# A five-group slot softmax, w2b loaded in pieces, seven homes for w1b and halved w2b work in the token loop of an attention and mixture-of-experts kernel

## The reference

```python
# retention attention: B, H, S, D = 4, 8, 768, 64
state = gamma * state + k_t v_t^T          # per head
y_t = q_t state / sqrt(D)                  # x = y as 3072 tokens x 512
# soft MoE: phi 512 x 32 (8 experts x 4 slots), w1 8 x 512 x 1024, w2 8 x 1024 x 512
logits = x @ phi
d = softmax(logits, over the 3072 tokens)  # slot softmax
slot_out[e] = relu((d.T @ x)[e] @ w1[e]) @ w2[e]
x = softmax(logits, over the 32 slots) @ slot_out
# top-2 MoE with noisy gates, 8 experts, w1 8 x 512 x 1024, w2 8 x 1024 x 512
top2 = the two largest of x @ w_gate + log1p(exp(x @ w_noise)) * noise
out = sum over the two experts of weight * (relu(x @ w1[e]) @ w2[e])
```

## Time and profile before

| what | value |
|---|---|
| runs | 612.53 us median of 3 (611.92, 612.53, 617.91) |
| the profiled execution | 616.65 us |
| its span on the core | 614.8 us |
| mean granted TensorE clock in it | 0.927 of full speed |
| busy: PE, PEld | 526.9 us (86%), 311.7 us (51%) |
| busy: DVE, ACT, POOL | 276.5 us (45%), 191.5 us (31%), 251.1 us (41%) |
| read from HBM, written to it | 93.87 MB, 29.70 MB |

### The profile page before, as it was taken

One profiled execution on the slowest core, in us unless ns is written; L12 is line 12 of the kernel. 1 busy time (PEld: TensorE's weight loads), 2 busy tenths in 40 slices (PEclk: granted clock), 3 DMA queues, 4 the chain that ended last, 5 costly groups with the idle time before them and its releaser, 6 DMA issues.

```text
span 614.8 us, 13368 instructions
## 1 busy us (share of the span) xinstructions
PE 526.9 (86%) x4842; PEld 311.7 (51%) x4843; DVE 276.5 (45%) x427; ACT 191.5 (31%) x349; POOL 251.1 (41%) x218
## 2 busy tenths in 40 slices
PE   4987989897875565567898999999999999999992
PEld 3866777775444542333444554555455445455451
DVE  2544646554553049883769323333332333332330
ACT  0121111222362043566695222222222222222120
POOL 1221212122010000234755766666666666666553
PEclk9998979999798656686999999999999999999997
DMA  7797897895999999883720222212232331433410
GB/s 236 261 314 277 301 321 250 307 346 205 333 378 385 388 408 405 333 324 98 289 71 22 55 51 50 44 38 48 42 52 48 47 53 24 52 49 42 52 18 1
DMA packets 48804, 107.88 MB, mean 175 GB/s; under 512 B 11482, under 2 KB 12746, under 8 KB 48769
## 3 DMA queue, kind: packets, MB, share of 16 engines
q1 hardware_dynamic: 34512, 92.89, 41.9%
q0 software_dynamic: 14256, 14.49, 13.6%
HBM read 93.87 MB, written 29.70 MB: 201 GB/s over the span
## 4 chain that ended last, share of the span: by engine, by line
PE 56%; DMA 15%; POOL 8%; issue 8%; DVE 6%; ACT 4%; SPq 0%; DVEq 0%; POOLq 0%; ACTq 0%
PE ps L859 30%; DMA w_region<-moe_w 5%; POOL out L537 4%; PE ps L570 4%; PE ps L614 4%; DMA s_region<-moe_w 3%; PE ps L609 3%; PE ps L842 3%; DMA w_region<-chunks 2%; PE ps L600 2%; POOL out L531 2%; DMA sw_region<-chunks 2%; POOL rec_region L525 2%; PE ps L714 2%; PE ps L621 2%
## 5 line engine op out<-in xcount | busy, mean ns | idle before, releaser
L859 PE MATMUL ps<-w_region,s_region 128*128 x1320 | 296.2, 381 | 1.2 <-ACT s_region L1033 1.2
L859 PEld LDWEIGHTS ps<-w_region,s_region 128*128 128x128 f16 x1320 | 127.5, 98 | 145.9 <-issue 4.8
L1432 DVE SCALAR_TENSOR_TENSOR s_region<-ps,s_region 128x1024 f16<-128x1024 f32 x55 | 67.3, 1224 | 186.3 <-ACT s_region L1033 186.3
L1033 ACT ACTIVATE s_region<-ps 128x1024 f16<-128x1024 f32 x55 | 56.2, 1023 | 71.3 <-PE ps L842 71.3
L537 POOL DMA_INDIRECT out<-s_region,rec_region x42 | 69.5, 1655 | 15.1 <-issue 12.2
L531 POOL DMA_INDIRECT out<-s_region,rec_region x42 | 47.4, 1128 | 65.7 <-DVE s_region L1446 65.4
L525 POOL DMA_INDIRECT rec_region<-records,idx x55 | 57.7, 1049 | 16.9 <-issue 16.9
L1023 ACT ACTIVATE s_region<-rec_region 128x128 f16 (+1 forms) x55 | 16.9, 307 | 129.9 <-DMA rec_region<-records,idx 129.9
L501 POOL PARTITION_ALL_REDUCE w2b_sum<-w2b_sum x8 | 8.4, 1053 | 82.6 <-ACT sw_region L953 55.9
L467 POOL TENSOR_TENSOR s_region<-w_region,s_region 128x512 f32<-128x512 f32 x14 | 15.0, 1070 | 64.2 <-DMA w_region<-chunks 45.8
L1446 DVE TENSOR_SCALAR s_region<-ps,rec_region,y_scale 128x512 f32<-128x512 f32 x42 | 33.8, 806 | 6.7 <-PE ps L859 4.0
...
## 6 DMA issues: line engine op xcount, KB each, us to landing
...
out<-s_region,rec_region POOLq DMA_INDIRECT x84, 2.8
```

The costliest lines, as they stand in the source:

```text
L859: last = nc.tensor.matmul(bank[6 + r], h[:, r, f, :], w2b_parts[:, bass.ds(e, 1), part, f, :].rearrange("p e m -> p (e m)"), start=(first ...
L1033: nc.scalar.activation(h_hi[:, r, :, :].rearrange("p c t -> p (c t)").rearrange("p (a n) -> p a n", a=2), ps[:, 2 + 2 * r:4 + 2 * r, :], A ...
L1432: nc.vector.scalar_tensor_tensor(out=h_lo[:, r, :, :].rearrange("p c t -> p (c t)").rearrange("p (a n) -> p a n", a=2), in0=ps[:, 2 + 2 * ...
```

## The change

- The slot softmax has NG = 5 groups of chunks: 0-3, 4-7, 8-13, 14-19 and 20-23. The first three are worked inside the attention, at chunks 7, 11 and 17. The fourth's products stand behind the last chunk, in PE's gaps while the last group's maximum is found. The last group has buffers of its own.
- w2b0 is loaded as three quarters (behind the last `keep_x_t`) and one quarter. w2b1 is loaded as two outer quarters (behind the fourth group's sums) and an inner half (behind the last group's).
- w1b2 goes to unit 7, and w1b now has homes in units 3 to 7 so that a load waits for an older product. w2b2 is loaded behind w1b1, w2b3 behind w1b3. w2b3 waits for `sw_product(2)`; w2b7 is loaded ahead of w2b6 and waits for w2b2's low part, w2b6 for w2b3's.
- `sw_product`s 1, 4 and 5 stand earlier on PE. On DVE the records' weights are computed behind the ranks, w2b2's scale stands later, and one low half stands ahead of the loop's last preparations where three stood. On POOL two fetches stand ahead of the second `sw_all_sum`.
- ACT makes w2b3's high part in two halves: one directly ahead of the loop, one behind `stage_c(2)`. In the loop, sums and high parts of w2b4 to w2b7 are dealt out in pieces; DVE's low parts of w2b2 (second half) and w2b3 stand behind tiles 0 and 1, of w2b4 to w2b7 behind tiles 2, 4, 5 and 6.

```diff
+    GROUPS = ((0, 4), (4, 8), (8, 14), (14, NT - REP), (NT - REP, NT))
...
-        w1b_home = [unit(u) for u in (6, 3, 4, 5, 6, 4, 5, 6)]
+        w1b_home = [unit(u) for u in (6, 3, 7, 4, 5, 6, 3, 4)]
...
                 elif e == 3:
-                    sp.wait_ge(w2b_lo_ready, 2)
+
+                    sp.wait_ge(ring_used, 2 * E + 3)
                 elif e < 6:
 
-                    sp.wait_ge(ring_used, 2 * E + e + 3)
+                    sp.wait_ge(ring_used, 2 * E + e + 1)
                 else:
-                    sp.wait_ge(w2b_lo_ready, 4)
+                    sp.wait_ge(w2b_lo_ready, {6: 4, 7: 3}[e])
...
+            sp.wait_ge(x_t_ready, NT)
+            load_w2b_quarters(0, 0, 3)
+            sp.wait_ge(slot_in_done, NG - 1)
+            load_w2b_quarters(1, 0, 1)
+            load_w2b_quarters(1, 3, 4)
+            sp.wait_ge(logits_kept, NT)
+            load_w2b_quarters(0, 3, 4)
+            sp.wait_ge(slot_in_done, NG)
+            load_w2b_quarters(1, 1, 3)
...
+            slot_sums(NG - 2, range(REP), bank[0], GROUPS[NG - 2][1])
+            turn_max(NG - 1)
+            slot_sums(NG - 2, range(REP, GROUPS[NG - 2][1] - GROUPS[NG - 2][0]), bank[0], GROUPS[NG - 2][1])
+            den_sums(NG - 2, NT)
+            spread_max(NG - 1)
+            slot_sums(NG - 1, range(REP), bank[1], NT)
...
+            w2b_high_half(3, 0)
...
-            w2b_low(2)
-            w2b_low(3, (0,))
+            w2b_low(2, (0,))
             sw_scales(1)
...
-                if i == 0:
-                    w2b_low(3, (1,))
+                if i < 2:
+                    w2b_low(*((2, (1,)), (3,))[i])
...
-                if i in (1, 3, 5, 6):
-                    w2b_low({1: 4, 3: 5, 5: 6, 6: 7}[i])
+                if i in (2, 4, 5, 6):
+                    w2b_low({2: 4, 4: 5, 5: 6, 6: 7}[i])
```

More of the change, by code:

```diff
@@ L578, in logit_parts_of @@
                     pe.wait_ge(logits_kept, b * NC + c)
-                if b > 0 and c == 3:
-                    pe.wait_ge(den_kept, b)
+                for g in group_ending(b * NC + c - 3):
+                    if g < NG - 2:
+                        pe.wait_ge(den_kept, g + 1)
                 for d in range(DC):
@@ L595, in turn_x @@
                     pe.wait_ge(x_kept, b * NC + c)
-                if b > 0 and c == 3:
-                    pe.wait_ge(slot_in_kept, b)
+                for g in group_ending(b * NC + c - 3):
+                    if g < NG - 2:
+                        pe.wait_ge(slot_in_kept, g + 1)
                 for d in range(DC):
@@ L802, in _ @@
             sw_product(0)
+            sw_product(1)
             pe.wait_ge(chosen_ready, 1)
@@ L812, in _ @@
             pe.wait_ge(ranks_read, 1)
+            sw_product(4)
             sort_rows(0)
@@ L816, in _ @@
             sw_spread_parts(1)
-            sw_product(4)
             sort_rows(1)
             sort_rows(2)
+            sw_product(5)
             sw_spread_parts(2)
             sw_spread_parts(3)
-            for e in range(5, E):
-                sw_product(e)
+            sw_product(6)
+            sw_product(7)
             for e in range(4, E):
@@ L946, in w2b_sums, with exp_slots @@
[L946 to L954 removed]
+            def exp_slots(g):
+                act.wait_ge(cols_shifted, g + 1)
+                if g > 0:
+                    nc.scalar.activation(fade[:, g:g + 1], max_all[:, g:g + 1], ACT.Exp, scale=-1.0,
+                                         bias=max_all[:, g - 1:g]).then_inc(fade_ready, 1)
+                nc.scalar.activation(exp_of(g), exp_of(g), ACT.Exp).then_inc(exp_cols_ready, 1)
@@ new lines, in keep_den @@
+            def keep_den(g):
+                act.wait_ge(den_done, g + 1)
+                nc.scalar.activation(den_part[:, g, :], bank[LG][:, 480:482], ACT.Copy).then_inc(den_kept, 1)
+            for t in range(NT):
+                keep_chunk(t)
+                for g in group_ending(t - 1):
+                    exp_slots(g)
+                for g in group_ending(t - 2):
+                    if g < NG - 2:
+                        keep_den(g)
+            keep_den(NG - 2)
+            exp_slots(NG - 1)
@@ new lines, in _, with w2b_high_half @@
+            keep_den(NG - 1)
+            def w2b_high_half(e, half):
+                if half == 0:
+                    act.wait_ge(w2b_scale_ready, e + 1)
+                    if e <= EARLY:
+                        act.wait_ge(ring_used, (4, 6, E + 5, 2 * E + 7, 3 * E)[e])
+                    else:
+                        act.wait_ge(w2b_lo_ready, e)
+                chunks = slice(half * FC // 2, (half + 1) * FC // 2)
+                nc.scalar.activation(w2b_parts[:, e, 0, chunks, :],
+                                     w2b_in[e].rearrange("p (c m) -> p c m", c=FC)[:, chunks, :],
+                                     ACT.Copy, scale=w2b_scale[:, 2, e:e + 1]).then_inc(w2b_hi_ready, 1)
@@ new lines, in w2b_high, with w2b_sum_part @@
+            def w2b_high(e):
+                for half in range(2):
+                    w2b_high_half(e, half)
+            def w2b_sum_part(e, part, unused):
+                parts, done = w2b_sum_parts(e), w2b_sums_of(e) + part
+                if part == 0:
+                    act.wait_ge(w2b_full[e], {0: 32, 1: 48}.get(e, 16))
+                if done > 0:
+                    act.wait_ge(w2b_sum_ready, done)
+                nc.scalar.activation(unused, w2b_in[e][:, part * UNIT // parts:(part + 1) * UNIT // parts], ACT.Abs,
+                                     accum_out=w2b_sum[:, 0, e, part:part + 1]).then_inc(w2b_sum_ready, 1)
@@ L956, in sw_sums @@
+            def w2b_sums(e, unused):
+                for part in range(w2b_sum_parts(e)):
+                    w2b_sum_part(e, part, unused)
             def sw_sums(e):
@@ L1389, in _ @@
             sw_scales(0)
+            w2b_scale_by_sum(2)
             by_lo = [P, LO_PART, P]
```

271 lines of the change are left out of this document (137 added, 134 removed).

## The result

| | before | after |
|---|---|---|
| median of the runs, us | 612.22 (610.51 to 617.91, 4 runs) | 624.11 (619.14 to 624.86, 4 runs) |
| ratio, 95% interval | | 1.0151 [1.0098, 1.0204] |
| profiled execution / its span | 616.65 / 614.8 | 624.86 / 623.1 |
| last product with w2a starts | 212.42 | 207.47 |
| loop's first product starts | 281.69 | 280.43 |

The change costs 1.5%. It was forecast at 614.0, no change. The weights' stream did come 5.0 us earlier, but the stretch from there to the loop became 3.7 us longer and the loop lost another 9.6.

What follows compares the result with a forecast made beforehand. The token loop was taken as the last bound, with the weights' stream holding the stages ahead. Of 4.4 us gained only 0.4 survived the late load; +1.9 behind it gave +1.5: 614.0 us against 612.53, range 608.5 to 619.0.

Steps and rivals of the forecast that it cites:

- Groups in attention: Attention's slot sums on PE: two groups need one round instead of two, gaining 1.0 us (0 to 1.9).
- The stream: Weight loads behind attention: w2b0 issued 1.8 us earlier, and 1.4 us of lost transfer rate recovered.
- Gating and folding: Stretch from the last w2a product towards the loop: 1.1 us more gained, bounds 0 and 3.
- Half high part ahead of `stage_c(0)`: Half of w2b3's high part on ACT directly ahead of the loop: costs 0.9 us (0 to 1.95).
- The loop's first tiles: w2b6 issued 8.1 us later in the loop, so its wait leaves only 0.4 of the 4.4 us gained.
- S': Start of the loop's first product in the changed kernel: forecast 277.3, 4.4 us earlier than before.
- Behind that: Tiles after the w2b6 wait: 2.0 us lost to crowded ACT, 1.7 to w2b7's wait, 1.8 saved: +1.9.
- The prediction's own sign of being wrong: Wrong if ACT's w2b6 sum doesn't wait for a DMA, the loop isn't 3 to 6 us earlier, or attention ends later.
- (a): Rival: the front ahead of the loop gains more, every bound at its good end: 611.1 us; chance 0.18.
- (d): Rival: the early loads bring nothing, as the queue's rate sets w2a's arrival: 617.2 us; chance 0.06.
- (b): Rival: the late w2b6 load holds nobody in the loop's first tiles: 606.5 us; chance 0.10.
- (c): Rival: slower because shorter slot sums leave attention's chunk loads uncovered: 620 us; chance 0.11.

Runs made afterwards that it cites:

- e4: e1 with ACT's high part of w2b2 moved behind four keeps: ratio 0.9934 to the kernel before.
- e1: Changed kernel with DVE's low parts early, w2b2's whole ahead of the loop and w2b3's behind tile 0: 616.01 us, ratio 1.0030 to the kernel before.
- e2: Changed kernel with w2b3's load issued behind w1b4 instead of w1b3: 622.22 us, ratio 1.0135 to the kernel before.
- a0: Control: the changed kernel with only one wait of PE written another way: 621.23 us, ratio 1.0111 to the kernel before.
- g2: g1 with w2b3's load issued behind that of w1b4: 605.57 us, ratio 0.9810 to the kernel before.
- b1: Kernel before with only the changed kernel's order of DVE's low parts of w2b2 and w2b3: ratio 1.0174 to the kernel before.
- e6: e1 with w2b2's high part behind four keeps, `sw_high` ahead of w2b3's sums, and the half high part behind `stage_c(2)`: ratio 0.9919 to the kernel before.
- e3: Changed kernel with both edits, w2b3's load behind w1b4 and the low parts of w2b2 and w2b3 early: 613.32 us, ratio 0.9987 to the kernel before.
- f1: e1 with w2b0 and w2b1 each loaded by one DMA instead of early pieces: 618.12 us, ratio 1.0029 to the kernel before.
- g1: e6 with both halves of w2b3's low part right behind `h_low(0)` on DVE: 606.82 us, ratio 0.9894 to the kernel before.
- e5: e1 with `sw_high` moved ahead of the sums of w2b3 on ACT: ratio 0.9976 to the kernel before.
- b0: Control: the kernel before with only one wait of PE written another way: ratio 1.0010 to the kernel before.

## Why the prediction was wrong, step by step

*Groups in attention*, 1.0 forecast. Attention ended 2.7 us earlier in the pair of profiles. But it ended at 148.45, 144.81 and 143.97 in three profiles with the old part and between 140.46 and 145.71 in twelve with the new one. The means differ by 2.1, less than either scatters: they point the forecast's way, but the gain isn't settled.

*The stream*, 1.8 + 1.4. From the end of attention to the last w2a product the old part took 63.1 to 64.1 us in three profiles, the new one 60.2 to 61.8 in eleven: 2.7 in place of 3.2. Right. The gap was closed only in part (273 GB/s from 156 to 162), because w2a's first load waits for its home and not for the queue: SP issues it at 158.36, as the product with w1a0 ends. Together the last w2a product came at 207.47, forecast 208.2.

*Gating and folding*, "-1.1" within 0 to 3. **This step failed first, by its sign.** The stretch to `sw_product(7)` grew by 2.9 us. That is no chance of one pair: it is 55.0 to 55.6 us in the three profiles with the old order, and 57.9 to 60.3 in the eight that keep both the changed part and the place of w2b3's load. I had asked "is w1b7 there?", and answered by ten units at the full 406 GB/s. I didn't ask whether SP would be allowed to issue them: the new wait of w2b3's load for `sw_product(2)` stands in front of the last four of w1b on SP and leaves the queue at 327 and 189 GB/s for 11 us. And I credited ACT with the pieces that it lost, not with those that it got: the high part of w2b2 now stands ahead of the keeps. The two costs lay beside each other. e4 took ACT's away and left the way to `sw_product(7)` at 58.0 (e1 58.2); e2 took the queue's away and left 57.1 (changed kernel 57.9, a0 60.3), because `sw_high` then stood behind the later w2b3; g2, with both gone, cut it by 4.4. And DVE's low parts, which I had counted among the pieces that leave this stretch, cost nothing there: b1 took two halves away and the loop started at the same time.

*Half high part ahead of `stage_c(0)`*, +0.9. From `sw_product(7)` to the loop it was 15.0 us, 14.3 before, with 1.8 of a stall that isn't its doing. e6 moved the half piece, and the same way took 11.7 us, but no run did that alone. Bounds kept, size open.

*The loop's first tiles.* The mechanism was right and is shown from both sides (e1, b1): issue forecast at S' + 19.8, measured 20.3; sum forecast to wait 7.6, measured 9.75. The mis-sized term is **the landing of a single load, 8.4 forecast, 10.9 measured** (10.2 to 10.3 in a0 and e2, 9.6 to 10.0 in e1, e3 to e6 and f1, 10.5 in g1). My rows were of loads into a quiet or a weights-only machine; here the records' fetches and the output rows run beside it, and in the changed kernel, a0 and e2 w2b7's load was issued only 7.8 us before. That one of these is the cause is my guess; no run was aimed at it, and g1's 10.5 came without w2b7's load beside it. The upper end of the range, 11.0, had it. The Trainium skill, DMA: Bandwidth & Descriptors, section Anatomy of one DMA, fits its fixed cost and its rate to transfers issued from GpSimd, and these are issued from SP; the estimate of 6.8 us by its figures lies further from every one of these loads than 8.4 does.

*Behind that*, 2.0 and 1.7 forecast, 1.59 and 1.67 measured: right. Not forecast was the lower clock behind the long wait, 1.5 us.

The prediction's own sign of being wrong came true: S' was to be 3 to 6 us earlier and is 1.3 earlier, and the stretches at 273, 327 and 189 GB/s lie under the 340 that it had named. The sum was +1.5, the profile has +8.3. Of the 6.8 between them 3.9 are the middle's (+3.7 for -0.2, and 1.8 of it is the stall below), 2.5 the turn's (33.5 us behind the loop's first product for 30.95), 1.5 the clock's, less 0.8 that the front gave in addition and 0.3 of the two small waits. Of the rivals, (a) and (d) fell: the front gained about what was forecast, no more and no less. (b) fell by the turn's wait. (c) named the right side with the wrong mechanism; attention never got slower. What I missed is a rival on the weights' queue: a new wait on SP in the middle of the stream.

## What to carry to other kernels

When a list of loads is re-ordered, check for each load what its queue waits for before it, and what stands behind it; bandwidth times bytes is only the time if nothing in front waits. An edit that tries out a suspected cost and brings nothing shows only that another chain is as long, or that the edit lengthened one itself: look at what now waits, and repeat it once that is cut (e2 against g2). And a piece of work whose end frees a home belongs as early as its engine has a gap, here 4.6 us of work in 6.2 us of idle time, which took 2.9 us off the span in one pair of profiles (e6 and g1; their ratios, 0.9919 and 0.9894, don't tell them apart by themselves).

## What the runs showed that wasn't expected

- The same wait gives two different tiles behind it. After PE waits of 8.79 to 10.34 us the next 24 products took 6.88 to 7.18 us in all four profiles. After 2.73 to 3.59 us they took 5.34 in four profiles (before, e3, e4, e6), but after 2.81 to 4.02 us 6.79 to 7.69 in four others (e1, e5, f1, b0), with the granted clock at 0.74 in e1's window from 302 to 308.5. A short wait can cost 1.5 to 2.3 us more than its length, and one profile doesn't tell whether it will.
- In eight of fifteen profiles PE's wait for `h_high(0)` ahead of the loop's first product was 2.4 to 4.6 us, in seven 0.8 to 1.2. The order of the instructions isn't what decides it: a0 and the changed kernel differ in one wait's form and show 1.20 and 2.98. ACT's idle time there is put down to nothing on this core ("remote"):

```profile
279.16 1.02 ACT L1092 ACTIVATE s_region<-ps 128x1024 f16<-128x1024 f32 x1 [2.96 <-remote]
```

  The products that it waits for had ended at 277.35. None of the three profiles of the kernel before and of b0 and b1 shows it. The cause stays open; no run was aimed at it.
- Attention's end scatters by 4.5 to 5.3 us between profiles with one and the same attention part, on a stretch of 145; in the one batch that holds both parts it is 144.81 and 143.97 against 142.81. A gain of a microsecond or two there can't be read from one pair of profiles.
